# Two buffers for layer one's weights and activations, low parts 192 bytes off step; layer two's odd inputs moved by 192 bytes

## The chip, the cores and the metric

The kernel runs on one core of one Trainium2 chip. The metric is the device time of one execution in microseconds (us). Three timed runs of the kernel before are shown; their median is 604.41 us (604.3 to 605.33).

## The reference

Attention first, then two feed-forward layers over the same 1536 tokens of 512 features:

```python
q, k, v: (2, 8, 768, 64)              # batch, heads, tokens, head size
scores = q @ k.T / 8, kept where the key is one of the first 4 ("sinks")
         or one of the last 128 up to the query; softmax; @ v
x = attention output as (1536, 512)
h = x @ w_in;  g = max(0.01*h, h);  x = g @ w_out        # layer one, 512 -> 2048 -> 512
h = x @ w_in2; g = h * sigmoid(h);  y = g @ w_out2       # layer two, 512 -> 2048 -> 512
```

## The kernel before

**The split.** All products are made to float32 accuracy from pairs of `float32r` numbers: a high part (ACT rounds the value on its way into the buffer) and a low part (DVE subtracts the high part from the raw value). A product is three matmuls, in the order `PASSES = ((HI, HI), (HI, LO), (LO, HI))`, where the first letter pair is the stationary operand (the weights that TensorE loads with a LDWEIGHTS of its own) and the second the moving one. Each matmul has its own weight load, and the load of the next matmul runs while the present one streams.

**Layer one** goes through 48 steps F: three blocks of 512 tokens, 16 slices of 128 hidden features in each. `hidden(F, half)` (L1307 to L1325) multiplies a slice of `w_in` (stationary, buffer `win`) with the block of x (moving): 12 matmuls of 512 columns in a step. ACT takes the result twice out of PSUM, once as float32 (L729) and once as the high part of `g` (L731), and `low_g` on DVE (L987) makes the low part. `project(F, half)` (L1327 to L1345) multiplies a slice of `w_out` (stationary, buffer `wout`) with `g` (moving): 12 more matmuls of 512 columns. The first 33 steps are interleaved with the attention of later tiles: score products of 260 columns (L1225), transposes of 128 columns (L1250, L1265) and products with the values (L1283, L1296) stand between the halves of `hidden` and `project`. The rest has TensorE for itself.

**Layer two** is 24 steps q, 8 for each block of 512 tokens. A step takes two slices of hidden features and makes their product with the block of the input in seven half-size products (Strassen's scheme, `strassen`, L1355): 42 matmuls of 256 columns at L1350, with the weight sums `w7_...` stationary and the input sums `xs_even` (blocks 0 and 2) or `xs_odd` (block 1) moving. Then `project_pair` (L1384) has 24 matmuls of 512 columns at L1399, in two trains of 12; there the roles are swapped: `g2` is stationary and `wout` moving. In each step a train of 12 projections stands after 30 matmuls of L1350, and another after 12.

**Order.** Each engine's instructions are written out by hand in one order; semaphores count how far the others are. The change touches no order and no wait.

**Where the buffers lie.** All buffers span 128 partitions, so a byte address within a partition says it all. Counted from the start of `w_raw` the kernel allocates, in this order: `w_raw` 16,384 bytes, `wout` 24,576, `g_f32` 4,096, `w7_even_low` 7,168, `x` 49,152, and at `one_at` (101,376, that is 99 times 1024) `win` (24,576) and `g` (8,192); at `one_end` `qk_raw` (12,480, that is 12 times 1024 plus 192), then the attention's buffers from `att_at` on. So modulo 1024, `x`, `win`, `wout` and `g` all begin at 0, high and low parts alike (in `win`, `wout` and `g` the low part is 2,048 or 4,096 bytes behind the high one; in `x` 24,576). A weight load takes 128 columns, 512 bytes, so it begins at 0 or at 512.
Layer two's buffers lie over those of layer one and of the attention by `over` (L206). `xs_even` is at `att_at`, 192 modulo 1024. `w7_odd_high` and `w7_even_high` are at 192, `w7_odd_low` and `w7_even_low` at 0: the high weights are in step with `xs_even`, the low ones begin 192 bytes before. `xs_odd` is at `one_at`, 0: in step with the low weights, and 192 bytes before the high ones. `qk_plain`, the raw input of the first attention tiles, lies over `win` and `g`, 16,384 bytes behind `one_at`.

Of the kernel before, what the change touches and what calls it, by code (L numbers as in the profile page):

```python
# [13 lines left out]
LOWEST = -8.0e9  # L14
START_MIN = 3.0e38


def sink_window_attention_two_ffn(
# [3 lines left out]
    TILES, _, HD = vt.shape  # L22
    D = qk.shape[2]
    H = HD // D
# [9 lines left out]
    QW = P + NS + P  # L34
    SCALE = 1.0 / float(D) ** 0.5
    REP = P // (H * NS)
    BLK = 512
# [3 lines left out]
    RAW = 3  # L41
    SPLIT = PLAIN - 1
    assert qk_first.shape[0] == PLAIN and qk.shape[0] == TILES - SPLIT
    assert D == 64 and HD == 512 and REP == 4 and window <= P and NS <= P and FT == 16 and TILES == 12 and TPB == 6

    KEPT = 6
    RING = 4
    QR = 3
# [21 lines left out]
    split_of, split_w, split_slot, slot_left, first_step = [], [], [], [], []  # L70
    resident, free = {}, [(s, -1) for s in range(KEPT)]
    for F, (b, f) in enumerate(steps):
        if f not in resident:
            slot, left = free.pop(0)
# [5 lines left out]
        j = resident[f]  # L80
# [6 lines left out]
    for q in range(NPF):  # L87
        for i in range(2):
            slot, left = free.pop(0)
# [13 lines left out]
    early_out = {7 + 4 * j: j for j in range(EARLY)}  # L103
# [48 lines left out]
    with ExitStack() as ctx:  # L152
        def sb(name, shape, dt):
            return ctx.enter_context(nc.sbuf_tensor(name, shape, dt))
# [12 lines left out]
        x_at = nc.sbuf_base  # L167
        x = sb("x", [P, 2, C, TILES * P], F32R)
        one_at = nc.sbuf_base
        win = sb("win", [P, KEPT, 2, HD], F32R)  # L170
        g = sb("g", [P, 2, 2, BLK], F32R)
        one_end = nc.sbuf_base

        qk_raw = sb("qk_raw", [P, QR, H // 2, QW], F32)
        att_at = nc.sbuf_base
# [30 lines left out]
        def over(at, *tensors):  # L206
            made = []
            for name, shape, dt in tensors:
                made.append(nc.alloc_sbuf_tensor_at(name, [P] + shape, dt, offset=at))
                at += 4 * prod(shape)  # L210
            return made, at


        (qk_plain,), end = over(one_at + 4 * 4 * 2 * HD, ("qk_plain", [RAW, H // 2, QW], F32))
        assert end <= one_end

        (y_f32, g2, c_sum, d_sum, e_sum), end = over(
            x_at, ("y_f32", [C, TILES * P], F32), ("g2", [2, 2, 4, 2 * P], F32R), ("c_sum", [2, 2 * P], F32),
            ("d_sum", [2 * P], F32), ("e_sum", [2 * P], F32))
        assert end <= one_at  # L220
        (xs_odd,), end = over(one_at, ("xs_odd", [7, 2, BLK], F32R))
        assert end <= one_end
        (stage,), _ = over(att_at + 4 * 14 * BLK, ("stage", [2, 2, 2, 2 * P], F32))
        (xs_even, w7_odd_high), end = over(
# [72 lines left out]
        def h_bank(F):  # L297
            return s_ps if F >= TWO_H and F % 2 == 0 else h_ps
# [16 lines left out]
        win_high, wout_high = sem("win_high"), sem("wout_high")  # L315
        win_ready, wout_ready = sem("win_ready"), sem("wout_ready")
# [17 lines left out]
        h_taken = sem("h_taken")  # L334
# [170 lines left out]
        def _(pool):  # L505
# [119 lines left out]
            def split_first(j, part, to, high, ready):  # L625
                pool.wait_ge(w_loaded[j % RING], 16)
                raw = w_raw[:, j % RING, part * HD:(part + 1) * HD]
                nc.gpsimd.tensor_copy(to[:, split_slot[j], 0, :], raw).then_inc(high, 1)
                pool.wait_ge(high, j + 1)
                nc.gpsimd.tensor_tensor(to[:, split_slot[j], 1, :], raw, to[:, split_slot[j], 0, :].bitcast(F32),  # L630
                                        ALU.subtract).then_inc(ready, 1)

            def sum_weights(q):
# [10 lines left out]
            for u in range(LAST):  # L644
                if u == FS - 1:
                    split_x(scaled_in[u])
                if u in inverted_in:
                    spread_inverse(inverted_in[u])
                if 2 * AHEAD < u <= NPAIR:
                    scale_pair(u - 1)  # L650
                for T, half in split_in(u - 1):
                    if not half and u - 1 > FS:
                        low_qk(T, half)
                if u % 2 == 0 and 0 < u <= NPAIR:
                    gather_sinks(u // 2 - 1)
                if u in scaled_in and u != FS - 1:
                    split_x(scaled_in[u])
                for T, half in split_in(u):
                    if half or u == FS:
                        low_qk(T, half)  # L660
                if u in early_in:
                    split_first(early_in[u], 0, win, win_high, win_ready)
                if u in early_out:
                    split_first(early_out[u], 1, wout, wout_high, wout_ready)
            for q in range(FP):
                sum_weights(q)

# [1 line left out]
        def _(act):  # L669
# [38 lines left out]
            def high_win(j):  # L708
                act.wait_ge(w_loaded[j % RING], 16 * (j // RING + 1))
                wait(act, h_done, slot_left[j] + 1)  # L710
                if j == EARLY:
                    act.wait_ge(win_high, EARLY)
                if 4 <= j < KEPT:
                    act.wait_ge(s_written, PLAIN * H)
                nc.scalar.activation(win[:, split_slot[j], 0, :], w_raw[:, j % RING, 0:HD],
                                     ACT.Copy).then_inc(win_high, 1)

            def high_wout(j):
# [7 lines left out]
            def take_hidden(F):  # L726
                act.wait_ge(h_done, F + 1)
                wait(act, g_ready, F - 1)
                nc.scalar.activation(g_f32[:, F % 2, :], h_bank(F)[:, :], ACT.Prelu, alpha=0.01)  # L729
                wait(act, y_done, F - 1)  # L730
                nc.scalar.activation(g[:, 0, F % 2, :], h_bank(F)[:, :], ACT.Prelu, alpha=0.01).then_inc(h_taken, 1)  # L731

            def evacuate(F, half):
                if F < 0 or F % FT != FT - 1:
# [66 lines left out]
            for a in range(LAST):  # L801
                head = a < FS
                F = a - FS
# [71 lines left out]
        def _(dve):  # L875
# [93 lines left out]
            def low_win(j):  # L969
                dve.wait_ge(win_high, j + 1)  # L970
                if j == EARLY:
                    dve.wait_ge(win_ready, EARLY)
                slot = split_slot[j]
                nc.vector.tensor_tensor(win[:, slot, 1, :], w_raw[:, j % RING, 0:HD],
                                        win[:, slot, 0, :].bitcast(F32), ALU.subtract).then_inc(win_ready, 1)

            def low_wout(j):
                dve.wait_ge(wout_high, j + 1)
# [5 lines left out]

            def low_g(F):
                dve.wait_ge(h_taken, F + 1)
                nc.vector.tensor_tensor(g[:, 1, F % 2, :], g_f32[:, F % 2, :], g[:, 0, F % 2, :].bitcast(F32),  # L987
                                        ALU.subtract).then_inc(g_ready, 1)

            def evacuate(F, half):  # L990
# [99 lines left out]
            for a in range(LAST):  # L1090
                head = a < FS
                F = a - FS
# [85 lines left out]
        @block.tensor  # L1178
        def _(pe):
            mm = nc.tensor.matmul  # L1180
            HI, LO = 0, 1
            PASSES = ((HI, HI), (HI, LO), (LO, HI))

            def fill(n):
# [122 lines left out]
            def hidden(F, half):  # L1307
                b, f = steps[F]
                if half == 0:
                    pe.wait_ge(win_ready, split_of[F] + 1)  # L1310
                    wait(pe, h_taken, F - 1 if F >= TWO_H else F)
                    if F == 0:
                        pe.wait_ge(s_read, S_FOUR)
                    if F == TWO_H:
                        pe.wait_ge(s_read, 2 * NPAIR)
                if F % FT == 0:

                    pe.wait_ge(x_ready, 2 * (b + 1) * TB - 1 + half)
                for c in (2 * half, 2 * half + 1):
                    for wp, xp in PASSES:  # L1320
                        ins = mm(h_bank(F)[:, :], win[:, split_slot[split_of[F]], wp, c * P:(c + 1) * P],  # L1321
                                 x[:, xp, c, tokens(F)],
                                 start=(c == 0 and wp == HI and xp == HI), stop=(c == C - 1 and wp == LO))
                if half == 1:
                    ins.then_inc(h_done, 1)  # L1325

            def project(F, half):  # L1327
                b, f = steps[F]
                first, last = F % FT == 0, F % FT == FT - 1
                if half == 0:  # L1330
                    pe.wait_ge(wout_ready, split_of[F] + 1)
                    pe.wait_ge(g_ready, F + 1)
                    if F == 0:
                        pe.wait_ge(s_read, S_TWO)
                        pe.wait_ge(pT_act, early("pair"))
                        pe.wait_ge(half_ready, early("half"))
                        pe.wait_ge(att_ready, E_EARLY)
                for d in (2 * half, 2 * half + 1):
                    if first and b:
                        pe.wait_ge((y_act, y_dve)[d % 2], 2 * (b - 1) + d // 2 + 1)  # L1340
                    for wp, gp in PASSES:
                        ins = mm(y_ps[d][:, :], wout[:, split_slot[split_of[F]], wp, d * P:(d + 1) * P],  # L1342
                                 g[:, gp, F % 2, :],
                                 start=(first and wp == HI and gp == HI), stop=(last and wp == LO))
                ins.then_inc((y_half, y_done)[half], 1)  # L1345

# [59 lines left out]
            for a in range(LAST):  # L1406
                F = a - FS
# [130 lines left out]
```

## Time and profile before

| | us |
|---|---|
| median of three timed runs | 604.41 |
| the profiled execution, its own time | 607.31 |
| its span | 605.6 |
| TensorE matmul busy | 599.2 (99%) |
| VectorE busy | 365.7 (60%) |
| ScalarE busy | 305.2 (50%) |
| GpSimd busy | 141.6 (23%) |

PE is TensorE's matmuls, PEld its weight loads, DVE VectorE, ACT ScalarE, POOL GpSimd. The start of a matmul is recorded, its end is modelled: a matmul of 512 columns is shown with some 389 ns and the next one begins long before that. Matmuls that follow each other on one line with the same tiles are merged in a timeline to one row, whose length runs from the first start to the last modelled end. What a matmul really costs is therefore read from starts: from one train's start to the next one's, divided by the matmuls between.

### The profile page before, as it was taken

What the parts mean: (1) busy time and instruction counts of PE and PEld (TensorE: products, weight loads), DVE (VectorE), ACT (ScalarE), POOL (GpSimd) and SP (SyncE); (2) the same over time, 40 slices, a digit from 0 to 9 for tenths busy, and PEclk for the clock granted to TensorE, in tenths of its full rate; (3) what the DMA queues carried; (4) which work ended last, traced back from release to release, by engine and by line L of the source; (5) the groups of instructions that cost most, each with busy time, mean ns of one, the idle gap of its engine ahead of it and who ended that gap; (6) DMA issues with size and microseconds to landing.
All of it is one profiled execution on the core that took longest, in us unless ns stands there. A gap on an engine that the chain in (4) does not pass through costs nothing.

```text
span 605.6 us, 10156 instructions
## 1 busy us (share of the span) xinstructions
PE 599.2 (99%) x3562; PEld 507.7 (84%) x3562; DVE 365.7 (60%) x808; ACT 305.2 (50%) x666; POOL 141.6 (23%) x194
## 2 busy tenths in 40 slices
PE   9999999999999999999999999999999999999997
PEld 4778888888788888888878899999898989999996
DVE  3864653545556667422784476766677675756562
ACT  5775555654436453223354464646555464645442
POOL 4934353343344251150575000000000000000000
PEclk9999999999999999999999999999999999999999
DMA  8623543526123222130786534353435544445301
GB/s 288 197 83 84 178 129 102 159 93 169 37 53 106 88 69 82 59 113 2 248 291 234 183 130 157 122 165 123 154 113 168 184 148 140 130 158 192 122 0 70
DMA packets 26961, 80.58 MB, mean 133 GB/s; under 512 B 3360, under 2 KB 4512, under 8 KB 26912
## 3 DMA queue, kind: packets, MB, share of 16 engines
q1 hardware_dynamic: 26912, 79.94, 41.4%
q8 instruction: 29, 0.48, 0.3%
q14 instruction: 20, 0.16, 0.1%
HBM read 71.54 MB, written 8.39 MB: 132 GB/s over the span
## 4 chain that ended last, share of the span: by engine, by line
PE 94%; DVE 3%; ACT 1%; issue 1%; DMA 1%; SPq 0%; ACTq 0%; DVEq 0%
PE y_ps L1399 22%; PE y_ps L1342 20%; PE h_ps L1321 17%; PE h_ps L1350 8%; PE s_ps L1350 8%; PE o_ps L1283 3%; PE t_ps L1350 3%; PE s_ps L1321 3%; PE s_ps L1225 2%; PE t_ps L1250 2%; PE y_ps L1211 1%; PE o_ps L1296 1%; PE s_ps L1211 1%; DVE x_sums L1019 1%; PE y_ps L1250 1%
## 5 line engine op out<-in xcount | busy, mean ns | idle before, releaser
L1342 PE MATMUL y_ps<-g,wout 128*128 128x512 f32 x576 | 146.8, 396 | 0.6 <-DVE g L987 0.6
L1399 PE MATMUL y_ps<-wout,g 128*128 128x512 f32 x576 | 138.9, 390 | 0.1
L1399 PEld LDWEIGHTS y_ps<-wout,g 128*128 128x128 f32 x576 | 104.8, 188 | 19.6 <-issue 0.5
L1342 PEld LDWEIGHTS y_ps<-g,wout 128*128 128x128 f32 x576 | 103.9, 188 | 20.6 <-issue 1.7
L1321 PE MATMUL h_ps<-x,win 128*128 128x512 f32 x480 | 118.6, 394 | 0.0
L1321 PEld LDWEIGHTS h_ps<-x,win 128*128 128x128 f32 x480 | 87.3, 188 | 17.4
L982 DVE TENSOR_TENSOR wout<-w_raw,wout 128x512 fp32r<-128x512 f32 x82 | 57.6, 703 | 46.1 <-ACT wout L723 46.1
L684 ACT ACTIVATE prob<-sm,neg_max 128x260 f32<-128x260 f32 (+2 forms) x96 | 42.8, 446 | 77.2 <-DVE sm L891 54.0
L786 ACT ACTIVATE g_f<-c_sum 128x512 f32<-128x512 f32 x24 | 15.2, 633 | 84.4 <-DVE c_sum L1040 84.4
L885 DVE CUSTOM_DVE_ANT_0 sm<-s_ps,mask 128x260 f32<-128x260 f32 (+1 forms) x67 | 27.3, 408 | 49.8 <-PE s_ps L1225 44.0
L987 DVE TENSOR_TENSOR g<-g_f,g 128x512 fp32r<-128x512 f32 x48 | 36.0, 750 | 32.7 <-ACT g L731 32.6
L729 ACT ACTIVATE g_f<-h_ps 128x512 f32<-128x512 f32 x40 | 23.8, 596 | 54.7 <-PE h_ps L1321 54.2
L723 ACT ACTIVATE wout<-w_raw 128x512 fp32r<-128x512 f32 x82 | 48.5, 620 | 0.0
L527 POOL TENSOR_TENSOR prob<-prob,row_inv 128x264 f32<-128x264 f32 (+2 forms) x28 | 19.2, 686 | 106.6 <-DVE row_inv L954 106.6
L1047 DVE TENSOR_TENSOR g<-g_f,g 128x512 fp32r<-128x512 f32 x48 | 33.0, 686 | 17.0 <-ACT g L775 15.8
L1350 PE MATMUL h_ps<-xs_even,w_even_high 128*128 128x256 f32 x192 | 35.2, 282 | 0.0
L1350 PE MATMUL s_ps<-xs_even,w_odd_high 128*128 128x256 f32 x192 | 35.0, 281 | 0.0
L1350 PEld LDWEIGHTS h_ps<-xs_even,w_even_high 128*128 128x128 f32 x192 | 30.3, 188 | 1.6 <-DVE e_sum L1034 0.3
L1350 PEld LDWEIGHTS s_ps<-xs_even,w_odd_high 128*128 128x128 f32 x192 | 30.5, 188 | 1.2
L1350 PE MATMUL h_ps<-xs_even,w_even_low 128*128 128x256 f32 x96 | 27.1, 282 | 0.0
L1350 PE MATMUL s_ps<-xs_even,w_odd_low 128*128 128x256 f32 x96 | 27.1, 282 | 0.0
L1225 PEld LDWEIGHTS s_ps<-k_hl,q_st 128*128 128x128 f32 x112 | 21.0, 188 | 5.2 <-issue 0.7
(159 smaller groups left out, 1012.2 us busy)
## 6 DMA issues: line engine op xcount, KB each, us to landing
w_sums<-w_sums SPq DMA_DIRECT2D x32, 640.0 KB, 3.9
w_raw<-w SPq DMA_DIRECT2D x36, 512.0 KB, 3.5
w_raw<-w SPq DMA_DIRECT2D x48, 384.0 KB, 3.1
qk_raw<-qk SPq DMA_DIRECT2D x28, 260.0 KB, 4.5
stage<-w SPq DMA_DIRECT2D x8, 512.0 KB, 5.6
v<-vt SPq DMA_DIRECT2D x12, 256.0 KB, 5.1
y<-qk_raw SPq DMA_DIRECT2D x12, 256.0 KB, 3.1
qk_plain<-qk_first SPq DMA_DIRECT2D x4, 520.0 KB, 3.4
```

What stands on the lines that cost most here:

```text
L684: nc.scalar.activation(prob[:, n % PR, 0:W], sm[:, n % 2, 0:W], ACT.Exp, scale=-1.0, bias=neg_max[:, n % 4:n % 4 + 1], accum_out=row_sum[: ...
L723: nc.scalar.activation(wout[:, split_slot[j], 0, :], w_raw[:, j % RING, HD:2 * HD], ACT.Copy).then_inc(wout_high, 1)
L729: nc.scalar.activation(g_f32[:, F % 2, :], h_bank(F)[:, :], ACT.Prelu, alpha=0.01)
L885: nc.vector.tensor_tensor_reduce(out=sm[:, n % 2, 0:W], in0=s_bank(n)[:, 0:W], in1=mask[:, v, 0:W], scale=-SCALE, scalar=START_MIN, op0=AL ...
L982: nc.vector.tensor_tensor(wout[:, slot, 1, :], w_raw[:, j % RING, HD:2 * HD], wout[:, slot, 0, :].bitcast(F32), ALU.subtract).then_inc(wou ...
L987: nc.vector.tensor_tensor(g[:, 1, F % 2, :], g_f32[:, F % 2, :], g[:, 0, F % 2, :].bitcast(F32), ALU.subtract).then_inc(g_ready, 1)
L1047: nc.vector.tensor_tensor(g2[:, q % 2, 1, part, :], g_f32[:, half, :].rearrange("p (i n) -> p i n", i=2), g2[:, q % 2, 0, part, :].bitcast ...
L1225: ins = mm(bank_[:, 0:W], q_st[:, h, :], k_hl[:, part, h, 0:W], start=part == HI, stop=part == LO)
L1321: ins = mm(h_bank(F)[:, :], win[:, split_slot[split_of[F]], wp, c * P:(c + 1) * P], x[:, xp, c, tokens(F)], start=(c == 0 and wp == HI and ...
L1342: ins = mm(y_ps[d][:, :], wout[:, split_slot[split_of[F]], wp, d * P:(d + 1) * P], g[:, gp, F % 2, :], start=(first and wp == HI and gp == ...
L1350: ins = mm(to, w_part(q, w_i, 1, wp)[:, 0, c * P:(c + 1) * P], x_part(q // FP, x_i, xp)[:, c, :], start=start and c == 0 and wp == HI and ...
L1399: ins = mm(y_ps[d][:, :], g2[:, q % 2, gp, at, d % 2 * P:(d % 2 + 1) * P], wout[:, slot, wp, :], start=(first and wp == HI and gp == HI), ...
```

## The change

`win` becomes `win_low` and `win_top`, `g` becomes `g_high` and `g_low`, with pieces of padding (`skip0` to `skip3`) between them. From `one_at` on the bytes are now: 832 of padding; `win_low` 12,288 (at 832 modulo 1024, so 192 bytes before a multiple of 1024); 192 of padding; `win_top` 12,288 (at 0); `g_high` 4,096 (at 0); 192 of padding; `g_low` 4,096 (at 192); 832 of padding. The region grows from 32,768 to 34,816 bytes, and what lies behind it keeps its place modulo 1024. `xs_odd` moves from `one_at` to `one_at + 192`. `qk_plain` now ends where `g_low` ends, and begins at 21,504 behind `one_at`, again 0 modulo 1024. The engines' instructions are the same in kind, number, shape and order; only addresses differ.

```diff
+    SHIFT = 192
...
-        win = sb("win", [P, KEPT, 2, HD], F32R)
-        g = sb("g", [P, 2, 2, BLK], F32R)
+        sb("skip0", [P, (1024 - SHIFT) // 4], F32)
+        win_low = sb("win_low", [P, KEPT, HD], F32R)
+        sb("skip1", [P, SHIFT // 4], F32)
+        win_top = sb("win_top", [P, KEPT, HD], F32R)
+        g_high = sb("g_high", [P, 2, BLK], F32R)
+        sb("skip2", [P, SHIFT // 4], F32)
+        g_low = sb("g_low", [P, 2, BLK], F32R)
+        plain_end = nc.sbuf_base
+        sb("skip3", [P, (1024 - SHIFT) // 4], F32)
         one_end = nc.sbuf_base
+        win, g = (win_top, win_low), (g_high, g_low)
...
-        (qk_plain,), end = over(one_at + 4 * 4 * 2 * HD, ("qk_plain", [RAW, H // 2, QW], F32))
-        assert end <= one_end
+        (qk_plain,), end = over(plain_end - 4 * RAW * H // 2 * QW, ("qk_plain", [RAW, H // 2, QW], F32))
+        assert end == plain_end
...
-        (xs_odd,), end = over(one_at, ("xs_odd", [7, 2, BLK], F32R))
+        (xs_odd,), end = over(one_at + SHIFT, ("xs_odd", [7, 2, BLK], F32R))
...
-                        ins = mm(h_bank(F)[:, :], win[:, split_slot[split_of[F]], wp, c * P:(c + 1) * P],
+                        ins = mm(h_bank(F)[:, :], win[wp][:, split_slot[split_of[F]], c * P:(c + 1) * P],
                                  x[:, xp, c, tokens(F)],
...
-                                 g[:, gp, F % 2, :],
+                                 g[gp][:, F % 2, :],
```

The same renaming is made at L628 and L630 (GpSimd's first two weight slices), L715 and L731 (ACT), L974 and L987 (DVE).

## Rows read from the trace of the kernel before

**Rows 1.** Page, parts 1 and 2: busy time of each engine, and the granted clock.

```profile
span 605.6 us, 10156 instructions
PE 599.2 (99%) x3562; PEld 507.7 (84%) x3562; DVE 365.7 (60%) x808; ACT 305.2 (50%) x666; POOL 141.6 (23%) x194
...
PEclk9999999999999999999999999999999999999999
```

**Rows 2.** Page, part 4: the chain that ended last, by engine.

```profile
PE 94%; DVE 3%; ACT 1%; issue 1%; DMA 1%; SPq 0%; ACTq 0%; DVEq 0%
```

**Rows 3.** Groups by line: count, busy us, mean ns, idle before and its releaser.

```profile
L1342 PE MATMUL y_ps<-g,wout 128*128 128x512 f32 x576 | 146.8, 396 | 0.6 <-DVE g L987 0.6
L1399 PE MATMUL y_ps<-wout,g 128*128 128x512 f32 x576 | 138.9, 390 | 0.1
L1321 PE MATMUL h_ps<-x,win 128*128 128x512 f32 x480 | 118.6, 394 | 0.0
...
L1321 PE MATMUL s_ps<-x,win 128*128 128x512 f32 x96 | 23.1, 389 | 0.0
```

**Rows 4.** Waits: who waited for whom, us in total, times, longest.

```profile
ACT g_f L729 <- PE h_ps L1321: 54.2, 31, 5.3
```

**Rows 5.** Timeline of PE in layer one without attention: start us, length us, train.

```profile
274.83 2.88 PE L1342 MATMUL y_ps<-g,wout 128*128 128x512 f32 x12
277.55 2.88 PE L1321 MATMUL h_ps<-x,win 128*128 128x512 f32 x12
280.27 2.88 PE L1342 MATMUL y_ps<-g,wout 128*128 128x512 f32 x12
...
307.47 2.88 PE L1342 MATMUL y_ps<-g,wout 128*128 128x512 f32 x12
```

**Rows 6.** Timeline of PE in layer two: projection trains five steps apart, blocks 0, 1, 2.

```profile
369.54 2.88 PE L1399 MATMUL y_ps<-wout,g 128*128 128x512 f32 x12
...
421.47 2.88 PE L1399 MATMUL y_ps<-wout,g 128*128 128x512 f32 x12
...
431.87 2.91 PE L1399 MATMUL y_ps<-wout,g 128*128 128x512 f32 x12
...
484.07 2.91 PE L1399 MATMUL y_ps<-wout,g 128*128 128x512 f32 x12
...
525.78 2.88 PE L1399 MATMUL y_ps<-wout,g 128*128 128x512 f32 x12
...
577.71 2.88 PE L1399 MATMUL y_ps<-wout,g 128*128 128x512 f32 x12
```

**Rows 7.** Weight loads of L1350: duration ns min/median/max, first and last start.

```profile
L1350 PEld LDWEIGHTS h_ps<-xs_even,w_even_high x192: 186/188/192, 349.7 to 585.6; 128*128 128x128 f32 x192
...
L1350 PEld LDWEIGHTS h_ps<-xs_even,w_even_low x96: 188/192/193, 350.0 to 585.7; 128*128 128x128 f32 x96
...
L1350 PEld LDWEIGHTS h_ps<-xs_odd,w_even_low x48: 187/188/189, 430.6 to 502.6; 128*128 128x128 f32 x48
```

**Rows 8.** Weight loads of L1321, and DVE making the low parts of `win`; same columns.

```profile
L1321 PEld LDWEIGHTS h_ps<-x,win x480: 187/188/193, 41.0 to 346.0; 128*128 128x128 f32 x160
...
L974 DVE TENSOR_TENSOR win<-w_raw,win x34: 674/682/1772, 45.0 to 333.1; 128x512 fp32r<-128x512 f32 x34
```

**Rows 9.** Timeline of PE in layer one among the attention's matmuls.

```profile
184.61 0.40 PE L1225 MATMUL s_ps<-k_hl,q_st 128*128 128x260 f32 x2
184.85 1.54 PE L1321 MATMUL h_ps<-x,win 128*128 128x512 f32 x6
186.23 0.27 PE L1265 MATMUL t_ps<-ident,prob_sink 128*128 128x128 f32 x1
186.26 1.63 PE L1321 MATMUL h_ps<-x,win 128*128 128x512 f32 x6
```

**Rows 10.** DVE making low parts of layer two's weight sums; columns as in rows 3.

```profile
L1004 DVE TENSOR_TENSOR w_odd_low<-w_sums,w_odd_high 128x512 fp32r<-128x512 f32 x12 | 8.2, 683 | 0.0
```

More of the change, by code:

```diff
@@ L14 @@
 LOWEST = -8.0e9
+HI, LO = 0, 1
 START_MIN = 3.0e38
@@ L627, in split_first @@
                 raw = w_raw[:, j % RING, part * HD:(part + 1) * HD]
-                nc.gpsimd.tensor_copy(to[:, split_slot[j], 0, :], raw).then_inc(high, 1)
+                nc.gpsimd.tensor_copy(to[HI][:, split_slot[j], :], raw).then_inc(high, 1)
                 pool.wait_ge(high, j + 1)
-                nc.gpsimd.tensor_tensor(to[:, split_slot[j], 1, :], raw, to[:, split_slot[j], 0, :].bitcast(F32),
+                nc.gpsimd.tensor_tensor(to[LO][:, split_slot[j], :], raw, to[HI][:, split_slot[j], :].bitcast(F32),
                                         ALU.subtract).then_inc(ready, 1)
@@ L663, in _ @@
                 if u in early_out:
-                    split_first(early_out[u], 1, wout, wout_high, wout_ready)
+                    split_first(early_out[u], 1, (wout[:, :, 0, :], wout[:, :, 1, :]), wout_high, wout_ready)
             for q in range(FP):
@@ L714, in high_win @@
                     act.wait_ge(s_written, PLAIN * H)
-                nc.scalar.activation(win[:, split_slot[j], 0, :], w_raw[:, j % RING, 0:HD],
+                nc.scalar.activation(win[HI][:, split_slot[j], :], w_raw[:, j % RING, 0:HD],
                                      ACT.Copy).then_inc(win_high, 1)
@@ L730, in take_hidden @@
                 wait(act, y_done, F - 1)
-                nc.scalar.activation(g[:, 0, F % 2, :], h_bank(F)[:, :], ACT.Prelu, alpha=0.01).then_inc(h_taken, 1)
+                nc.scalar.activation(g[HI][:, F % 2, :], h_bank(F)[:, :], ACT.Prelu, alpha=0.01).then_inc(h_taken, 1)
             def evacuate(F, half):
@@ L973, in low_win @@
                 slot = split_slot[j]
-                nc.vector.tensor_tensor(win[:, slot, 1, :], w_raw[:, j % RING, 0:HD],
-                                        win[:, slot, 0, :].bitcast(F32), ALU.subtract).then_inc(win_ready, 1)
+                nc.vector.tensor_tensor(win[LO][:, slot, :], w_raw[:, j % RING, 0:HD],
+                                        win[HI][:, slot, :].bitcast(F32), ALU.subtract).then_inc(win_ready, 1)
             def low_wout(j):
@@ L986, in low_g @@
                 dve.wait_ge(h_taken, F + 1)
-                nc.vector.tensor_tensor(g[:, 1, F % 2, :], g_f32[:, F % 2, :], g[:, 0, F % 2, :].bitcast(F32),
+                nc.vector.tensor_tensor(g[LO][:, F % 2, :], g_f32[:, F % 2, :], g[HI][:, F % 2, :].bitcast(F32),
                                         ALU.subtract).then_inc(g_ready, 1)
@@ L1180, in _ @@
             mm = nc.tensor.matmul
-            HI, LO = 0, 1
             PASSES = ((HI, HI), (HI, LO), (LO, HI))
```

## The prediction

> **What bounds the kernel now.** I read the page's busy times first. TensorE's matmuls are busy for 599.2 of 605.6 us, at the full granted clock in every slice, the 2.4 GHz level; DVE is at 60%, ACT at 50% [rows 1]. The chain that ended last is TensorE for 94% [rows 2]. Three lines of 512-column matmuls make up most of it: 576 at L1342, 576 at L1399 and 480 + 96 at L1321, with almost no idle time before them [rows 3]. The change adds and removes no instruction, so it can only act through the time that one instruction takes, and it matters on TensorE alone, since ACT waits for TensorE in layer one (54.2 us in 31 waits at L729) and not the other way round [rows 4]. Durations of matmuls are modelled, so I measure by starts, in the timeline.
>
> In layer one without attention the trains of 12 start 2.72 us apart without exception, from 274.83 to 307.47, 12 trains: 32.64 us for 144 matmuls, 226.7 ns each [rows 5]. 512 columns at 2.4 GHz would be 213.3 ns, so 13.3 ns of each matmul are something other than its columns. In layer two the same 12-matmul train is shown with 2.88 us in blocks 0 and 2 and with 2.91 in block 1. Five steps take 421.47 - 369.54 = 51.93 us in block 0, 577.71 - 525.78 = 51.93 in block 2 and 484.07 - 431.87 = 52.20 in block 1 [rows 6]. The code of the three blocks is the same but for the buffer of the input sums: `xs_even` begins in step (modulo 1024) with the high weights, `xs_odd` 192 bytes before them. So this trace already holds a trial of one part of the change.
>
> **The change part by part.**
>
> *`xs_odd` in step.* Block 1 then has exactly the relations of blocks 0 and 2: high weights in step with the input, low weights 192 bytes before. A step is worth (52.20 - 51.93) / 5 = 0.054 us; eight steps, 0.43 us. All of it is on the path, because TensorE is the end of every chain there and no engine limits block 1 other than it limits block 0. Bounds: starts are rounded to 0.01 us, so five steps are off by 0.02 at most and eight by 0.03; the gain is 0.40 to 0.46 us if the cause is the address, and 0 if block 1 is slower for another reason. I take 0.43, since block 2 returns to the value of block 0 to the last digit.
>
> *Low weights and low activations of layer one.* What changes is one weight load in three: while the matmul (HI, LO) streams the low x or the low g, the low weights of (LO, HI) are loaded. The load began in step with the stream (0 against 0, or 512 against 0), and now begins 192 bytes before: `win_low` at 832 against x at 0, and `wout`'s low part at 0 against `g_low` at 192. That is the relation that low weights have to `xs_even`. The other two loads of each product are high weights beside a high stream, and those addresses stay as they were modulo 1024. 576 matmuls at L1342 and 576 at L1321 make 1152 [rows 3], so 384 loads are touched. The trace has no 512-column matmul with that relation. Upper bound of the gain: all 13.3 ns go for those 384, 5.1 us. Upper bound of the loss, by the nearest row: something like block 1's penalty comes over layer one. That penalty shows as 0.03 us in each train of projections (2.91 against 2.88) [rows 6]; layer one has some 135 trains (about 108 up to 272 us, and 27 behind it), so 4.1 us. Within these I take 0, for two reasons. First, three different pairs of buffers, x with `win`, `g` with `wout`, and in layer two `wout` with `g2` in swapped roles, all have a train of 2.88 us [rows 5, 6]; a collision between the two streams would have to be the same in all three to the last digit, while a cost that each 512-column matmul has anyway is the simple reading. Second, in layer two the load with this relation is not faster: 192 ns median for `w_even_low` beside `xs_even`, against 188 beside `xs_odd`, and 188 for the high weights and for layer one's [rows 7, 8]. Beside a stream of 512 columns, 426 ns for two matmuls, 4 ns of a load are hidden; beside 256 columns they are hidden too, because there the blocks with the 192 ns loads are the faster ones.
>
> *Trains among the attention.* A train of six has 5 starts and a last modelled length: 5 x 0.2267 + 0.389 = 1.52 us. Behind two score matmuls it takes 1.54, behind a transpose 1.63 [rows 9]. Such tails are where block 1's penalty also sits, so here the layout might give or cost some 0.02 us for each of about 108 trains, 2 us either way. It is inside the bounds above; I take 0.
>
> *DVE, ACT and GpSimd.* They write and read the moved buffers. Subtracting a low part takes 682 ns in the median where all three operands are in step (`win`), and 683 ns in the mean where the result is 192 bytes off the two inputs (`w_odd_low`) [rows 8, 10]. So no cost. If each of the 34 + 48 subtractions took 10 ns more, ACT's waits of 54.2 us [rows 4] show the slack that covers it; without it, 0.8 us. `qk_plain` keeps its place modulo 1024 and its size. It now lies over `win_top`'s last two slots and `g`; slots 4 and 5 were the ones that waited for the end of the plain scores, so that wait is as before. No semaphore, transfer or queue is moved.
>
> *Sum.* -0.43 + 0 + 0 + 0. Of the profiled execution's own 607.31 us (its span is 605.6) this leaves 606.88. That execution was 2.90 us above the median of 604.41; the difference goes on the median: 604.41 - 0.43 = 603.98, say **604.0 us**.
>
> **A rule against the change.** The trace says that 192 bytes on the input's start are worth 0.054 us in a step [rows 6]. The Trainium skill, "SBUF — State Buffer", section "SBUF: two separate sides", holds that TensorE has its own ports, two independent ones for reading, and never waits on anyone; the addresses of two streams would then not matter at all. By that rule this change is worth 0 in both layers, 604.4 us. The difference between blocks speaks against it here, though only by 0.5% of a step. Its page "TensorE: Matmul & The Clock Gate", section "Back-to-back issue gap", gives 512/2.4 + 2.5, an estimate of 216 ns for a 512-column matmul. The trace shows 226.7; if the 10.7 ns between were collisions, the 384 touched ones would give back up to 4.1 us. No run here shows such a gap for this type.
>
> **The rivals.**
>
> *R1, layer one's streams do collide.* Part of the 13.3 ns is the weight load getting in the way of the stream, and the offset takes some of it away. For it: block 1 shows that relations cost something, and the same offset of low weights stands in layer two's faster blocks. Against it: the flat 2.88 in three pairs of buffers, and the 192 ns loads. The size, if relations matter in layer one as much for a matmul as in layer two: 0.054 us over 42 matmuls of L1350 is 1.27 ns, times 1152 is 1.5 us; 604.41 - 0.43 - 1.5 = 602.5. With half of the 13.3 ns on the 384 it would be 2.6 us, 601.4; with all of it 5.1, 598.9. In the stretch with attention a part would be lost again in waits for DVE's `g`.
>
> *R2, being out of step costs (slower).* In block 1 most loads are out of step, and it is the slow block. Layer one is now all in step and flat; after the change a third of its loads is not. If each train then pays block 1's 0.03 us, 135 x 0.03 = 4.1 us, and with -0.43 the time is 608.1. It decides from 0.012 us a train on (1.6 us, 605.6). For it: the longer loads [rows 7]. Against it: blocks 0 and 2 have exactly this third out of step and pay nothing, and their trains are 2.88.
>
> *R3, addresses don't do it.* Block 1 is slow for another reason and stays so: 604.4.
>
> **How the numbers follow.** No change but block 1 (604.0, its own range 603.3 to 604.8): 0.42. R1: 0.33, from 603.2 down to 599. R2: 0.14, from 605.6 to 608.1. R3: 0.11. What a measurement of this kernel can tell is about 0.2%, 1.2 us: faster means under 603.2, slower over 605.6. R1 is on the faster side nearly always, the forecast and R3 within; a small part of R1 and R2 falls within as well. Faster 0.32, same 0.55, slower 0.13. The range leaves out the deeper half of R1's tail and the upper part of R2: 601.6 to 605.9.
>
> **What would show it.** Block 1's trains at 2.88 us and five of its steps at 51.93 show the first part right; 2.91 would mean R3. Layer one's trains 2.72 us apart and 2.88 long mean that the offset does nothing there; starts closer than 2.72 are R1, wider ones R2. The first weight loads of `win_low` at 192 instead of 188 ns would show that the relation was carried over and is hidden. The trains among the attention should stay at 1.54 and 1.63. The forecast is wrong if the quiet stretch changes at all: 0.01 us in a train's distance there is 1 us over layer one.

## The result and the profile after

The changed kernel takes 606.53 us (median of nine runs, 605.81 to 609.79), the one before 604.49 (nine runs, 604.30 to 605.64): ratio 1.0033, interval 1.002 to 1.0047. It is slower by some 2 us where I had forecast 0.4 less.

The page of the kernel after: TensorE is as busy as before and is now 98% of the chain that ended last.

```profile
span 605.1 us, 10156 instructions
PE 599.3 (99%) x3562; PEld 507.1 (84%) x3562; DVE 366.6 (61%) x808; ACT 305.1 (50%) x666; POOL 141.9 (23%) x194
...
PE 98%; DVE 1%; issue 0%; ACT 0%; DVEq 0%; ACTq 0%
```

Its span, 605.1, is under the 605.6 of the trace before. Both traces have to be cut into stages to see why, and the timeline's starts do that. First, layer one without attention, where `hidden`'s train begins each step (start us, length us; trains are broken up now because `win_top` and `win_low` are two names):

```profile
276.94 0.63 PE L1332 MATMUL h_ps<-x,win_top 128*128 128x512 f32 x2
282.48 0.63 PE L1332 MATMUL s_ps<-x,win_top 128*128 128x512 f32 x2
288.03 0.63 PE L1332 MATMUL h_ps<-x,win_top 128*128 128x512 f32 x2
...
310.22 0.63 PE L1332 MATMUL h_ps<-x,win_top 128*128 128x512 f32 x2
...
315.76 0.63 PE L1332 MATMUL s_ps<-x,win_top 128*128 128x512 f32 x2
```

Seven steps from 276.94 to 315.76 take 38.82 us, 5.546 each, where two trains of 2.72 made 5.440 [rows 5]. That is 0.107 us more in each step, and as regular as the value before. Eight loads of a step are of the touched kind, so the cost is 13.3 ns for each of them on average.

Block 1 of layer two, two projection trains five steps apart:

```profile
431.77 2.88 PE L1410 MATMUL y_ps<-wout,g 128*128 128x512 f32 x12
...
483.70 2.88 PE L1410 MATMUL y_ps<-wout,g 128*128 128x512 f32 x12
```

51.93 us and a length of 2.88: exactly what blocks 0 and 2 had, where block 1 was at 52.20 and 2.91 [rows 6]. This half of the change works as forecast.

The stretch with attention, from the first `hidden` to that of step 33, first the kernel before, then the one after:

```profile
41.03 1.17 PE L1321 MATMUL h_ps<-x,win 128*128 128x512 f32 x4
...
266.65 0.61 PE L1321 MATMUL h_ps<-x,win 128*128 128x512 f32 x2
```

```profile
39.71 0.71 PE L1332 MATMUL h_ps<-x,win_top 128*128 128x512 f32 x2
...
265.84 0.62 PE L1332 MATMUL h_ps<-x,win_top 128*128 128x512 f32 x2
```

225.62 us became 226.13: 0.51 more.

**What differs by chance.** The two traces begin their first `hidden` 1.32 us apart, and the one before has a delay of its own at 313.65, where TensorE waited 0.57 us for `g`:

```profile
313.65 3.00 PE L1342 MATMUL y_ps<-g,wout 128*128 128x512 f32 x12 [0.57 <-DVE g L987]
```

Neither belongs to the layout: the trace of `odd_only` below, a kernel with the old layer one, has its first `hidden` at 39.52 and no such delay. Its stages begin here (first `hidden`, `hidden` of step 33, first matmul of layer two), and the changed kernel's layer two begins at 349.04:

```profile
39.52 0.71 PE L1321 MATMUL h_ps<-x,win 128*128 128x512 f32 x2
...
265.14 0.62 PE L1321 MATMUL h_ps<-x,win 128*128 128x512 f32 x2
...
346.74 0.40 PE L1350 MATMUL t_ps<-xs_even,w_even_high 128*128 128x256 f32 x2
```

```profile
349.04 0.40 PE L1361 MATMUL t_ps<-xs_even,w_even_high 128*128 128x256 f32 x2
```

Against that trace (span 602.8) the changed kernel's is 2.3 us longer: 0.19 before the first `hidden`, 0.51 in the stretch with attention, 1.60 in the rest of layer one (83.20 against 81.60 us), 0.00 in layer two. Layer two, from its first matmul to the start of its last, took 252.81 us before and takes 252.35 after: block 1 gave 0.46 us. The change as a whole is 2.11 - 0.46 = 1.65 us by the traces, inside the measured 1.2 to 2.8.

Loads and subtractions of `win_low` (duration ns min/median/max, first and last start) have the medians of before, 188 and 682 ns [rows 8], within 2 ns:

```profile
L1332 PEld LDWEIGHTS h_ps<-x,win_low x160: 187/188/192, 40.0 to 345.8; 128*128 128x128 f32 x160
...
L986 DVE TENSOR_TENSOR win_low<-w_raw,win_top x34: 673/684/1780, 43.7 to 332.7; 128x512 fp32r<-128x512 f32 x34
```

### The profile page after: what moved, and what is told of

Read it like the earlier page. It is cut to its first block, busy times and chain, and to the rows that moved or that the text cites. A ratio compares the mean times of both kernels' runs of the same rounds, so it can differ in the third digit from the quotient of the medians.

```text
span 605.1 us, 10156 instructions
## 1 busy us (share of the span) xinstructions
PE 599.3 (99%) x3562; PEld 507.1 (84%) x3562; DVE 366.6 (61%) x808; ACT 305.1 (50%) x666; POOL 141.9 (23%) x194
## 4 chain that ended last, share of the span: by engine, by line
PE 98%; DVE 1%; issue 0%; ACT 0%; DVEq 0%; ACTq 0%
PE y_ps L1353 22%; PE y_ps L1410 22%; PE h_ps L1332 18%; PE h_ps L1361 8%; PE s_ps L1361 8%; PE s_ps L1332 4%; PE o_ps L1294 3%; PE t_ps L1361 3%; PE s_ps L1236 2%; PE t_ps L1261 2%; PE y_ps L1222 1%; PE s_ps L1222 1%; PE o_ps L1307 1%; PE y_ps L1198 1%; PE y_ps L1261 1%; PE y_ps L1294 0%
## 5 line engine op out<-in xcount | busy, mean ns | idle before, releaser
L1353 PE MATMUL y_ps<-g_high,wout 128*128 128x512 f32 x384 | 134.1, 398 | 0.0
L1332 PE MATMUL h_ps<-x,win_top 128*128 128x512 f32 x320 | 101.1, 397 | 0.0
L1353 PEld LDWEIGHTS y_ps<-g_high,wout 128*128 128x128 f32 x384 | 72.1, 188 | 14.8 <-issue 0.7
L1353 PE MATMUL y_ps<-g_low,wout 128*128 128x512 f32 x192 | 75.5, 393 | 0.0
L1332 PEld LDWEIGHTS h_ps<-x,win_top 128*128 128x128 f32 x320 | 57.2, 188 | 11.4
L1332 PE MATMUL h_ps<-x,win_low 128*128 128x512 f32 x160 | 63.1, 395 | 0.0
L999 DVE TENSOR_TENSOR g_low<-g_f,g_high 128x512 fp32r<-128x512 f32 x48 | 35.2, 733 | 33.6 <-ACT g_high L743 33.4
L1059 DVE TENSOR_TENSOR g<-g_f,g 128x512 fp32r<-128x512 f32 x48 | 33.0, 687 | 16.7 <-ACT g L787 15.5
L1353 PEld LDWEIGHTS y_ps<-g_low,wout 128*128 128x128 f32 x192 | 36.2, 188 | 5.7
L1332 PEld LDWEIGHTS h_ps<-x,win_low 128*128 128x128 f32 x160 | 30.0, 188 | 6.8
```

What stands on the lines that cost most here:

```text
L999: nc.vector.tensor_tensor(g[LO][:, F % 2, :], g_f32[:, F % 2, :], g[HI][:, F % 2, :].bitcast(F32), ALU.subtract).then_inc(g_ready, 1)
L1059: nc.vector.tensor_tensor(g2[:, q % 2, 1, part, :], g_f32[:, half, :].rearrange("p (i n) -> p i n", i=2), g2[:, q % 2, 0, part, :].bitcast ...
L1332: ins = mm(h_bank(F)[:, :], win[wp][:, split_slot[split_of[F]], c * P:(c + 1) * P], x[:, xp, c, tokens(F)], start=(c == 0 and wp == HI and ...
```

## The experiments

Offsets below are in bytes from the start of the moving operand, x or the input sums, to the start of the weights. "A step" in layer one is one of the steps without attention (24 matmuls of 512 columns).

### One part alone

`odd_only`: the kernel before with one line of the change.

```diff
-        (xs_odd,), end = over(one_at, ("xs_odd", [7, 2, BLK], F32R))
+        (xs_odd,), end = over(one_at + 192, ("xs_odd", [7, 2, BLK], F32R))
```

> The kernel before with one line changed: xs_odd begins at one_at + 192. Theory A (each part of the change acts by itself: block 1 gains, layer one's offset costs): block 1's projection trains 2.88 us instead of 2.91, five of its steps 51.93 us instead of 52.20, layer one's quiet trains stay 2.72 us apart; time 0.43 us below before, ratio 0.9993. Theory B (the time of the changed kernel comes from something that all its parts share, such as the larger region): block 1 gains nothing by this line alone, ratio 1.000.

Measured: 604.22 us (12 runs) against 606.55 for the kernel before on the same chip (17 runs), ratio 0.9975, interval 0.9958 to 0.9992. Neither sign nor size can be taken from these medians: times come in two groups some 2 us apart, which go with the clock at the start (see below), and 10 of the 17 runs of the kernel before fell in the longer one, but only 1 of the 12. In the shorter group the medians are 604.39 and 604.15. Sign and size come from the trace. Block 1's trains:

```profile
429.47 2.88 PE L1399 MATMUL y_ps<-wout,g 128*128 128x512 f32 x12
...
481.41 2.88 PE L1399 MATMUL y_ps<-wout,g 128*128 128x512 f32 x12
```

Five steps in 51.94, so theory A; the gain in layer two is 0.46 us, and layer one is at 5.44 a step.

`win_only`: the changed kernel with `g` and `xs_odd` as before.

```diff
-        sb("skip2", [P, SHIFT // 4], F32)
         g_low = sb("g_low", [P, 2, BLK], F32R)
...
-        (xs_odd,), end = over(one_at + SHIFT, ("xs_odd", [7, 2, BLK], F32R))
+        (xs_odd,), end = over(one_at, ("xs_odd", [7, 2, BLK], F32R))
```

> The changed kernel with only the weights of layer one split and win_low 192 bytes before the step; g_high and g_low side by side and in step, xs_odd where it was. Theory A, with a price of 13.3 ns for each low load that is out of step beside a 512-column stream: hidden's trains of 12 take 2.773 us, project's 2.72, a quiet step of 24 matmuls 5.49 us. Rival (the cost hangs on the loads of wout beside g_low alone): step 5.44. Block 1 stays at 52.20 us in five steps.

`g_only`: the changed kernel with `win_low` in step and `xs_odd` as before.

```diff
-        sb("skip0", [P, (1024 - SHIFT) // 4], F32)
+        sb("skip0", [P, 1024 // 4], F32)
...
-        sb("skip1", [P, SHIFT // 4], F32)
```

> The changed kernel with only g_low 192 bytes behind the step; win_low and win_top in step, xs_odd where it was. Theory A: project's trains of 12 take 2.773 us, hidden's 2.72, a quiet step 5.49 us. Rival (the cost hangs on win_low alone): step 5.44. If both this and the other part give 5.55 or both 5.44, the price is not one for each out-of-step load.

First rows of `hidden` in successive steps, `win_only`:

```profile
278.62 0.61 PE L1331 MATMUL h_ps<-x,win_top 128*128 128x512 f32 x2
...
284.12 0.61 PE L1331 MATMUL s_ps<-x,win_top 128*128 128x512 f32 x2
...
289.62 0.61 PE L1331 MATMUL h_ps<-x,win_top 128*128 128x512 f32 x2
```

and `g_only`:

```profile
281.40 0.62 PE L1331 MATMUL s_ps<-x,win_top 128*128 128x512 f32 x2
...
286.92 0.62 PE L1331 MATMUL h_ps<-x,win_top 128*128 128x512 f32 x2
...
292.44 0.62 PE L1331 MATMUL s_ps<-x,win_top 128*128 128x512 f32 x2
```

5.50 and 5.52 us a step: each part costs by itself, 0.060 and 0.080, more than the 0.053 expected, and together (0.107) they cost less than the sum of the two. So theory A holds in kind, but its price of 13.3 ns a load is an average, not a constant: `win_low` alone costs 15 ns a load and `g_low` alone 20. The cost does not stay in its own train either. `win_only`'s untouched `project` trains take 2.731 us from start to start, `g_only`'s untouched `hidden` trains 2.760. In `win_only` the weights moved and in `g_only` the stream did, so it is the relation of the two that costs, not the place of one of them. The single times were 608.29 and 605.82 us; their first `hidden` came at 41.49 and 39.02 us, 2.47 us apart, as much as the times. Over the attention's stretch `win_only` lost 0.50 us and `g_only` 0.24.

### Layer two's low weights in step

```diff
-        (w7_odd_low,), end = over(end + 832, ("w7_odd_low", [7, 2 * P], F32R))
+        (w7_odd_low,), end = over(end, ("w7_odd_low", [7, 2 * P], F32R))
```

(with the pad behind it taken out too, and `xs_odd` at `one_at + 192`.)

> xs_odd moved by 192 as in the change, layer one as before, and w7_odd_low put in step with w7_odd_high and the input sums (it was 192 bytes before them); w7_even_low stays out of step, so that even steps q are the control within the run. If being in step is always cheapest: odd steps q take less than 10.387 us, 14 low loads x 13.3 ns = up to 0.19 us less each. If the offset helps beside streams of 256 columns, as its use there suggests: odd steps take longer than 10.387 us, by 0.05 us or more.

Two steps, an odd and an even one, from train to train:

```profile
371.93 2.88 PE L1399 MATMUL y_ps<-wout,g 128*128 128x512 f32 x12
...
392.86 2.88 PE L1399 MATMUL y_ps<-wout,g 128*128 128x512 f32 x12
```

20.93 us instead of 20.77 (twice 51.93 / 5). If the even steps stayed at 10.39, an odd one takes 10.54, and its 14 low loads cost 11 ns more each in step than out of step. That is the opposite of layer one: among the 256-column streams of layer two the offset helps, among the 512-column streams of layer one it hurts. The width is the plainest difference between the two, but no run varied it alone. The single time of 611.0 us holds three things: layer two 1.9 us longer than in `odd_only`, a first `hidden` 1.85 us later, and a delay of 2.8 us in the rest of layer one. There many of DVE's operations of 0.69 us took 1.0 to 1.8 us, in a stretch in which GpSimd was summing weights, and TensorE waited for `g`. The kernel before has such a delay too (at 313.65). Only the first is the edit's.

### Maps of the offset

Each step of layer one uses one of six slots of `win`. With another offset for each slot, one run shows six prices. `map1` to `map3` move the low part only (in layer two they also move the odd steps' low weights and `xs_odd`, as the expectations say):

```diff
-        win_low = sb("win_low", [P, KEPT, HD], F32R)
+        LOW_AT = [0, 64, 128, 192, 256, 320]          # map1; map2 384 ... 704; map3 16, 32, 768 ... 960
+        for slot, at in enumerate(LOW_AT):
+            gap = (at - (nc.sbuf_base - one_at)) % 1024
...
+            low_slots.append(sb(f"win_low{slot}", [P, HD], F32R))
```

> win_low in six pieces, one for each slot, that begin 0, 64, 128, 192, 256 and 320 bytes past a multiple of 1024; win_top, g_high, g_low and wout in step, so that a quiet step of layer one shows the price of its slot's offset (in step 5.440 us, 832 gave 5.500). Theory C (what counts is how far the load lies ahead of the stream modulo 1024, and only some distances collide): steps differ by slot, some at 5.440. Rival D (any low part out of step costs the same): slot 0 5.440, all others 5.500. Layer two: w7_odd_low 64 bytes before the high part (was 192): if it is enough to be out of step, odd steps q of block 0 stay at 10.387 us; if the distance counts, they lie between 10.387 and 10.544. xs_odd at 256, so the high weights begin 64 bytes before the input: by C block 1 gets faster than 10.387, by D slower, like the 10.440 of before.

> The same with offsets 384, 448, 512, 576, 640 and 704 for the slots of win_low. Theory C: steps differ by slot, and 512 (half a period away) is one of the free ones at 5.440. Rival D: all six 5.500. Layer two: w7_odd_low 384 bytes before the high part, xs_odd at 64, so that the high weights begin 128 bytes behind the input: by C block 1 lies between 10.387 and 10.544; by D at 10.440.

> The same with offsets 16, 32, 768, 832, 896 and 960. 832 (slot 3) must show 5.500 again. Theory C: 768 to 960 differ from each other. Rival D: all 5.500. Layer two: w7_odd_low 192 bytes behind the high part instead of before it (by C slower than 10.387 in block 0, by D the same), and xs_odd at 384, so that the high weights begin 192 bytes before the input and the low ones of even steps 384 before: if a load that begins before the stream is free, block 1's steps are the fastest of all, under 10.387, by up to 28 loads x 11 ns = 0.3 us.

First matmuls of the steps 33 to 39 in `map1`, slots 1, 2, 3, 4, 5, 0, 1:

```profile
265.15 0.39 PE L1344 MATMUL h_ps<-x,win_top 128*128 128x512 f32 x1
...
270.65 0.39 PE L1344 MATMUL s_ps<-x,win_top 128*128 128x512 f32 x1
...
276.15 0.39 PE L1344 MATMUL h_ps<-x,win_top 128*128 128x512 f32 x1
...
281.64 0.39 PE L1344 MATMUL s_ps<-x,win_top 128*128 128x512 f32 x1
...
287.08 0.39 PE L1344 MATMUL h_ps<-x,win_top 128*128 128x512 f32 x1
...
292.58 0.39 PE L1344 MATMUL s_ps<-x,win_top 128*128 128x512 f32 x1
...
298.02 0.39 PE L1344 MATMUL h_ps<-x,win_top 128*128 128x512 f32 x1
```

Offsets 64, 128 and 192 give steps of 5.50, 5.50 and 5.49 by these rounded starts, offset 256 gives 5.44, 320 gives 5.50 and 0 gives 5.44. All three maps together, by unrounded starts:

| low part's offset in layer one | step us |
|---|---|
| 0, 256, 512, 768 | 5.44 |
| 64, 320, 576, 832 | 5.50 |
| 128, 384, 640, 896 | 5.49 |
| 192, 448, 704, 960 | 5.49 |
| 32 | 5.52 |

(The piece meant for 16 is taken to have been put at 32 too; its step is the same 5.52.) The period is 256 bytes, not 1024. Theory C is right in that distances repeat, and rival D in that all but the distances of a whole period cost nearly the same. Layer two repeats with 256 as well: with high weights in step, two steps of block 0 take 20.77 us with the odd low weights at 64 (that is -192), 20.93 at 0, 20.88 at 128 (`map2`), and 20.82 both at -64 (`map1`) and at +192 (`map3`), which are one place modulo 256. Where one step of layer two is given a time below, it runs from its first matmul of 256 columns to that of the next step. In block 1 `map1`'s odd steps take 10.38 and `map2`'s 10.46, on theory C's side of 10.387 both times, though `map1`'s by a hair. `map3`'s guess for block 1, that weights before the input are free, was wrong: its steps take 10.44 and 10.49. Single times: 605.73, 607.41 and 606.28 us.

`map4` moves high and low part of a slot together, `map5` the high part alone, `map6` sets the low part 64 behind the high one; block 2 of layer two gets an input buffer of its own. The odd steps' low weights move as well: in step with the high ones in `map4`, 128 bytes behind them in `map5`, 64 before them in `map6`.

```diff
-        (xs_odd,), end = over(one_at, ("xs_odd", [7, 2, BLK], F32R))
+        (xs_odd,), end = over(one_at + Y, ("xs_odd", [7, 2, BLK], F32R))   # Y 64, 128, 32
...
+        (xs_last,), _ = over(att_at + Z, ("xs_last", [7, 2, BLK], F32R))   # Z 64, 64, 128
...
-            return (xs_even, xs_odd)[b % 2][:, i, part, :].rearrange("p (c n) -> p c n", c=2)
+            return (xs_even, xs_odd, xs_last)[b][:, i, part, :].rearrange("p (c n) -> p c n", c=2)
```

> From the kernel before. Layer one: high and low part of each win slot moved together, by 0, 64, 128, 192, 16 and 32 bytes (modulo 256) from x; g as before. Theory E (the relation of the load to the stream counts, with a period of 256 bytes, and 512-column streams are fastest in step): slot 0 shows a step of 5.440 us, all others more than the 5.500 that a displaced low part alone costs, since three loads in three are displaced. Rival F (the relation of low to high part counts): all steps 5.440. Layer two, with w7_odd_low in step with w7_odd_high: block 0 odd steps must repeat 10.544 us; block 1 (input 128 bytes before both parts) and block 2 (input 64 bytes behind both): by F 10.544 in all three blocks, by E another value in each; known so far for high and low relation in bytes modulo 256: (0, 64) 10.387, (192, 128) 10.383.

> From the kernel before. Layer one: only the high part of each win slot moved, by 0, 64, 128, 192, 16 and 32 bytes from x, low parts in step. Theory E: slot 0 5.440 us, the others dearer than with a displaced low part (5.493 to 5.520), as two loads in three are displaced. Rival F: the same prices as for a displaced low part. Layer two: relations to the input (high, low) of odd steps (64, 192) in block 1 and (192, 64) in block 2, which were not seen yet; open, 10.38 to 10.49 by the neighbours.

> From the kernel before. Layer one: win's high part at p and low part at p + 64 (modulo 256), p = 64, 128, 192, 0 ... in the order of the slots 64, 128, 192, 256, 336, 352. The slot with the high part in step shows 5.500 us as the changed kernel's part did; the others more by theory E, 5.500 by rival F. Layer two: odd steps with (high, low) of (128, 64) in block 2 and (160, 96) in block 1; open, a value under 10.383 us would point to a layout that beats both kernels.

(In `map6` the list of positions is that of the low parts; the high ones lie 64 before.) Steps of layer one:

| high part at | high and low together (`map4`) | high alone (`map5`) | low 64 behind high (`map6`) |
|---|---|---|---|
| 0 | 5.44 | 5.44 | 5.50 |
| 64 | 5.55 | 5.55 | 5.51 |
| 128 | 5.55 | 5.53 | 5.56 |
| 192 | 5.48 | 5.48 | 5.48 |

The main point of theory E holds in layer one: in step is the best. F falls, since high and low parts moved together are dear. But the price isn't that of the loads out of step added up, as E had it: at 192 a step costs 5.48 with all three loads moved and 5.49 with the low one alone, where E asked for more than 5.50. In layer two the odd steps of `map4` take 10.54 us in block 0 (in step) and 10.54 in block 1 (both parts at 128), where E expected different values, and 10.44 in block 2 (both at 192). `map6`'s new pairs were no better than the known ones: 10.53 for (160, 96), high and low, and 10.41 for (128, 64). `map5` had the find. In its block 1, with odd steps' high weights at 64 and low weights at 192, two steps go from

```profile
442.19 2.88 PE L1421 MATMUL y_ps<-wout,g 128*128 128x512 f32 x12
...
462.91 2.88 PE L1421 MATMUL y_ps<-wout,g 128*128 128x512 f32 x12
```

20.72 us, though the even steps there, at (64, 128), take 10.47; the odd ones take 10.25. In block 2, (192, 64) takes 10.29. Single times: 608.20, 606.40 and 608.35 us.

`map7` looked for a pair in layer one that beats in step, and for better neighbours of (64, 192), with Y 96 and Z 224.

> From the kernel before. Layer one: high and low part of the slots of win at (64, 192), (192, 64), (128, 64), (192, 128), (96, 224) and (32, 160) bytes modulo 256 from x. If 512-column streams have a cheaper relation than in step, a slot shows a step under 5.440 us; by theory E with in step as the best, all six are over 5.50. Layer two: odd steps with (96, 224) in block 1 and (32, 160) in block 2, the neighbours of (64, 192) at half the grid; between 10.20 and 10.40 if the price changes smoothly.

Layer one's six pairs take 5.51 to 5.54 us (slots with (192, 64), (128, 64), (192, 128), (96, 224), (32, 160) and (64, 192)): nothing beats 5.44 there. In layer two (96, 224) takes 10.43 and (32, 160) 10.47: the good place is narrow; the smooth change that was half expected would have kept both under 10.40. The time was 607.12 us.

### A version that beats both

`best1`: layer one all in step, layer two's weights at (64, 192) in all blocks.

```diff
+        sb("skip0", [P, 32], F32)
         w7_even_low = sb("w7_even_low", [P, 7, 2 * P], F32R)
+        sb("skip1", [P, 32], F32)
...
-        (xs_odd,), end = over(one_at, ("xs_odd", [7, 2, BLK], F32R))
+        (xs_odd,), end = over(one_at + 192, ("xs_odd", [7, 2, BLK], F32R))
...
+        (w7_odd_high,), end = over(end + 64, ("w7_odd_high", [7, 2 * P], F32R))
...
-        (w7_odd_low,), end = over(end + 832, ("w7_odd_low", [7, 2 * P], F32R))
+        (w7_odd_low,), end = over(end + 128, ("w7_odd_low", [7, 2 * P], F32R))
...
-            end + 192, ("w_sums", [2, 5, 2 * P], F32), ("x_sums", [2, 2 * P], F32),
+            end + 128, ("w_sums", [2, 5, 2 * P], F32), ("x_sums", [2, 2 * P], F32),
```

> The kernel before with layer one untouched (all in step) and layer two's high weights 64 bytes and low weights 192 bytes behind the input in all three blocks and for even and odd steps, the relation that gave 10.248 us a step in one run. Theory E (only these two relations modulo 256 count): all 24 steps at 10.25 us, so 8 x 0.19 + 16 x 0.14 = 3.8 us less than before, 600.7 us, ratio 0.9937. Rival (the 10.248 hung on something else in that run, such as the other step's addresses): steps of 10.38 or more, ratio 0.999.

```profile
368.60 2.90 PE L1401 MATMUL y_ps<-wout,g 128*128 128x512 f32 x12
...
389.18 2.90 PE L1401 MATMUL y_ps<-wout,g 128*128 128x512 f32 x12
```

Two steps in 20.58 us, 10.29 each, and so it stays through all three blocks: between the 10.25 that I had taken for the value and the rival's 10.38. So the forecast of 3.8 us was too high. The 10.25 of `map5` was partly a matter of where the step is cut: from projection train to projection train the same two steps take 10.30 and 10.42 instead of 10.25 and 10.47, so a part of a step's cost shows in the next one. Layer two takes 250.17 us instead of 252.81 in the trace before, 2.64 less. Measured: 604.11 us (12 runs, 601.75 to 604.57) against 604.65 for the kernel before (17 runs, 604.42 to 606.92), ratio 0.9975, interval 0.9961 to 0.9988. It beats the kernel before, and with it the changed one. The medians show less than the traces because of the clock at the start.

**The clock at the start.** Of the times beside this one, the kernel before has 14 between 604.4 and 605.7 us and 3 between 606.7 and 607.0; `best1` has 3 between 601.7 and 602.3 and 9 between 603.9 and 604.6. Group by group, `best1` is 2.7 us faster. The groups go with the moment at which TensorE's clock rises. The same three fill matmuls and the next two transposes in `odd_only`, whose first `hidden` began at 39.52, and in `best1`, where it began at 41.20:

```profile
6.78 0.81 PE L1187 MATMUL y_ps<-filler 128*128 128x512 bf16 x3
...
7.95 0.44 PE L1250 MATMUL y_ps<-ident,prob 128*128 128x128 f32 x2
```

```profile
7.42 1.49 PE L1189 MATMUL y_ps<-filler 128*128 128x512 bf16 x3
...
9.56 0.52 PE L1252 MATMUL y_ps<-ident,prob 128*128 128x128 f32 x2
```

0.81 us is the 2.4 GHz level (two spacings of 0.22 and a last length), 1.49 the 1.2 GHz level (two spacings of 0.43), though the page grants the full clock from the start in both. What TensorE did before was the same work in both. The fourteen traces bear this out: the four in which these fill matmuls are 0.43 us apart (`before`, `win_only`, `l2_in_step`, `best1`) have their first `hidden` at 41.0 to 41.5 us, the ten others at 38.8 to 39.7. So the trace of the kernel before, which I had read as full speed in every slice, ran slow for its first 8 us and more. That (1.51 us against `odd_only`) and the delay at 313.65 (0.85 us) are most of the 2.90 us that the prediction left unexplained. I have not tried what sets the moment; whether `best1` falls into the longer group more often for a reason is open.

## Why the prediction was wrong

**Block 1 in step: right.** 0.43 us forecast, 0.46 in the traces of the change and of `odd_only`, with 51.93 and 51.94 for five steps where 51.93 was named.

**Low weights and activations of layer one: the step that failed.** "Within these I take 0" was wrong: the offset costs 1.60 us in the stretch without attention, 13.3 ns for each of 120 touched loads. (That the 226.7 ns of a matmul also lie 13.3 above 213.3 is a coincidence as far as the runs show: the parts alone cost 15 and 20.) The bound had been drawn (4.1 us of loss), the value hadn't. Both reasons for 0 were poor. The first, the same 2.88 in three pairs of buffers, showed that a relation of 0 modulo 256 costs the same in all; all three pairs had that relation, and so none bore on another one. The second, the 192 ns loads, was no sign either way: `win_low`'s loads kept 188 ns, not the 192 that I had named as the mark of the relation, and the step still got longer. And the argument from layer two, that blocks 0 and 2 have this relation and pay nothing, compared them with block 1 and never with the state in step. `l2_in_step` made that comparison: in step is worse there and better in layer one. The range ended at 605.9 because I left out the upper part of R2.

**R2** has the sign, the place and, for layer one, the cause: out of step costs. Its price was wrong. I had it as block 1's penalty for each train, 0.03 us, 4.1 in all. It was 0.053 for each train of 12 in the stretch without attention and far less among the attention, 2.11 in all. (In R1's price, 0.054 us over 42 matmuls is 1.29 ns, not 1.27; the 1.5 us stay.) **R1** had the sign wrong. **R3** is refuted by block 1.

**Trains among the attention: 0 forecast, +0.51 us measured.** There are 33 steps with 8 touched loads, 264; at 13.3 ns they would cost 3.5 us. Six sevenths of it are missing. The traces show where the 0.51 us lie, in `hidden` alone: its matmuls that follow each other there are 235.0 ns apart on average where they were 233.5 in `odd_only`, and `project`'s stayed at 238.0 and 237.9. Both were above the 226.7 of the quiet stretch before the change, so part of the cost may have been paid already; that is not shown.

**DVE, ACT, GpSimd: right.** 684 ns against 682 for the low part of `win` [rows 8].

**The rules of the Trainium skill.** "SBUF — State Buffer", section "SBUF: two separate sides", with two independent read ports for TensorE, would make all layouts equal. Layer one's maps contradict that: 5.44 to 5.56 us for the same step by addresses alone. What inside the chip makes it so, no run shows. The 216 ns of "TensorE: Matmul & The Clock Gate" (section "Back-to-back issue gap") are what the bf16 fill matmuls of 512 columns take at the full clock (6.78, 7.00, 7.21 us in `odd_only`). The float32r trains of 512 columns didn't reach them in any layout; 226.7 stayed the least.

## What to carry to other kernels

Where TensorE is the bound and matmul starts are perfectly regular, read the spacing to the nanosecond and try the layout: where weights begin against the stream was worth 1% of layer two (2.64 of 252.8 us) and 2% of a step of layer one (0.107 of 5.44). The place that was good in one stage was bad in the other, so don't carry an offset from one stage to the next; give each of several interchangeable slots its own offset and let one trace show all the prices. And take differences by stage in the trace, because the moment at which the clock rises moved the time by some 2 us, no less than the edit.

## What the runs showed of the hardware

- Addresses of the stationary and the moving operand act on the matmul spacing with a period of 256 bytes within a partition. Beside 512 columns: 5.44 us for 24 matmuls at distance 0, 5.49 to 5.52 with only the low part elsewhere, up to 5.56 with the high part elsewhere too. In layer two's steps, whose loads lie beside 256 columns: low weights at 0, 64, 128, 192 with high ones in step: 20.93, 20.77, 20.88, 20.82 us for an odd and an even step (even ones at 64 throughout).
- The cost doesn't stay with the trains whose operands are out of step: `win_only` slowed the untouched `project` trains by 0.011 us, `g_only` the untouched `hidden` trains by 0.040.
- The recorded length of a weight load doesn't show it: 188 ns in the median with and without the cost.
- TensorE's clock went from the 1.2 to the 2.4 GHz level at different times in executions of like work: fill matmuls were already 0.22 us apart from 6.78 us on in `odd_only` and still 0.43 apart from 7.42 on in `best1`, while the granted clock was shown as full.
